# A convolution and MLP kernel whose opening is put in another order, with three accumulating transfers per tile in place of four

## The reference

```python
w = weight_gen - np.max(weight_gen, axis=-1, keepdims=True)
w = np.exp(w)
w = w / (np.sum(w, axis=-1, keepdims=True) + 1e-09)
x_pad = np.concatenate([np.zeros((B, pad, D), dtype=np.float32), x], axis=1)   # pad = 6
idx = np.arange(S)[:, None] + np.arange(K)[None, :]                            # K = 7
x_unf = x_pad[:, idx, :].reshape(B, S, K, H, group)                            # group = 24
out = np.einsum('bshk,bskhg->bshg', w, x_unf)                                  # 16384 x 192
h = out @ w_in                                                                 # 192 x 2048
g = np.maximum(0.01 * h, h)
return (g @ w_out).astype(np.float32)                                          # 2048 x 192
```

## Time and profile before

| | |
|---|---|
| median of 3 runs | 1037.89 us (1037.78 to 1038.11) |
| the profiled execution, its own time | 1039.72 us |
| its span, first to last instruction | 1037.9 us |
| PE busy with matmuls | 1026.1 us, 99% |
| DVE busy | 933.7 us, 90% |
| ACT busy | 634.8 us, 61% |
| POOL busy | 554.7 us, 53% |
| TensorE's granted clock, mean over the span | 0.997 |

### The profile page before, as it was taken

How to read it: one execution, slowest core, us unless ns; L and a number is a source line. 1 busy time by engine, 2 the same in 40 slices (tenths; PEclk the granted TensorE clock), 3 DMA queues, 4 the chain that set the end, 5 groups by cost and what they waited for, 6 DMA issues and landing times.

```text
span 1037.9 us, 28985 instructions
## 1 busy us (share of the span) xinstructions
PE 1026.1 (99%) x12761; PEld 673.6 (65%) x12761; DVE 933.7 (90%) x1196; ACT 634.8 (61%) x1352; POOL 554.7 (53%) x377
## 2 busy tenths in 40 slices
PE   9899999899999999999999999999999999999998
PEld 4566556466666666666666666666666666666667
DVE  7979999969999999999999999999999999998611
ACT  7866566465565665566565566565566565566554
POOL 0114556456566566556556556556556556556543
PEclk9999999999999999999999999999999999999999
DMA  9441212111131210312102121110312102111100
GB/s 265 102 99 32 81 35 97 34 32 66 35 96 35 59 66 8 97 35 97 34 17 81 35 97 34 50 66 17 97 34 97 34 18 81 34 35 35 34 17 17
DMA packets 68597, 60.62 MB, mean 58 GB/s; under 512 B 56380, under 2 KB 60732, under 8 KB 66488
## 3 DMA queue, kind: packets, MB, share of 16 engines
q1 hardware_dynamic: 67196, 55.35, 18.2%
q0 software_dynamic: 1152, 3.15, 1.7%
q10 hardware_dynamic: 124, 0.29, 0.1%
HBM read 29.34 MB, written 12.58 MB: 40 GB/s over the span
## 4 chain that ended last, share of the span: by engine, by line
PE 94%; DMA 2%; DVE 2%; SPq 1%; issue 0%; ACT 0%; POOL 0%; DVEq 0%; POOLq 0%
PE h_ps L1061 45%; PE t_ps L1171 23%; PE out_ps L1171 23%; PE out_ps L1125 1%; PE h_ps L1043 1%; PE out_ps L1135 1%; DMA rawD<-in_moe_w_in_dram 1%; SPq L383 1%; DMA conv<-prod 0%; DVE gl L883 0%; DMA prod<-prod 0%; SPq L386 0%; DVE prod L683 0%; PE h_ps L1099 0%; ACT gh L483 0%
## 5 line engine op out<-in xcount | busy, mean ns | idle before, releaser
L352 POOL TENSOR_TENSOR gl<-g,gh 128x512 f16<-128x512 f32 x360 | 545.6, 1542 | 413.3 <-ACT g L485 413.3
L483 ACT ACTIVATE gh<-h_ps 128x512 f16<-128x512 f32 x512 | 317.6, 620 | 373.8 <-PE h_ps L1061 362.3
L1171 PE MATMUL t_ps<-wo,gh 64*128 64x384 f16 (+1 forms) x1984 | 387.8, 318 | 4.3 <-issue 4.3
L1171 PE MATMUL out_ps<-wo,gh 64*128 64x384 f16 (+1 forms) x1984 | 387.8, 318 | 0.0
L1061 PE MATMUL h_ps<-xT,whA 64*128 64x512 f16 x1920 | 377.6, 376 | 0.0
L485 ACT ACTIVATE g<-h_ps 128x512 f32<-128x512 f32 x512 | 321.9, 629 | 0.0
L683 DVE TENSOR_TENSOR prod<-xbuf,taps 128x768 f32<-128x768 f32 x186 | 273.3, 1485 | 0.0
L697 DVE TENSOR_TENSOR conv<-conv,prod 128x768 f32<-128x768 f32 x174 | 264.5, 1520 | 1.0
L1171 PE MATMUL out_ps<-wo,gl 64*128 64x192 f16 x1920 | 233.4, 243 | 0.0
L1171 PE MATMUL t_ps<-wo,gl 64*128 64x192 f16 x1920 | 233.4, 243 | 0.0
L1171 PEld LDWEIGHTS t_ps<-wo,gh 64*128 64x128 f16 x1984 | 181.8, 94 | 51.6 <-issue 5.0
(11 more groups left out here) (111 smaller groups left out, 717.5 us busy)
## 6 DMA issues: line engine op xcount, KB each, us to landing
xbuf<-in_x_dram SPq DMA_DIRECT2D x15, 1344.0 KB, 6.0
out_dram<-stage SPq DMA_DIRECT2D x31, 384.0 KB, 2.3
taps<-in_weight_gen_dram SPq DMA_DIRECT2D x16, 224.0 KB, 5.9
xT_again<-xT SPq DMA_DIRECT2D x29, 64.0 KB, 2.1
rawO<-in_moe_w_out_dram SPq DMA_DIRECT2D x4, 384.0 KB, 9.9
conv<-prod POOLq DMA_DIRECT2D x4, 384.0 KB, 4.6
prod<-prod POOLq DMA_DIRECT2D x4, 384.0 KB, 4.4
rawA<-in_moe_w_in_dram SPq DMA_DIRECT2D x2, 512.0 KB, 8.2
```

The source lines that it names most:

```text
L352: nc.gpsimd.tensor_tensor(gl[:, q % RING, :], g[:, q % RING, :], gh[:, q % RING, :], ALU.subtract).then_inc(s_gl_p, 1)
L483: nc.scalar.activation(gh[:, q % RING, :], h_ps[q % GROUP][:], ACT.Prelu, alpha=SLOPE, scale=SHRINK0 if n < 2 * NG else SHRINK).then_inc(s ...
L1171: ins = nc.tensor.matmul(dst, a[rows, (m * NF + f) % RING, j * P:(j + 1) * P], moved, start=i == 0 and k < 2 and a is gh and f == 0 and pa ...
```

## The change

It consists of five edits.

1. **PE's opening.** `sum0` now collects in `out_ps` and `t2_ps` and the warm-up matmuls write an h bank. There are 15 + 4 of them in place of 16 + 5 + 4 + 4. The transposes of tile 0's hi follow directly on `spread_top(0)`; those of its lo stand inside `hidden_by_pe(0)`, behind the first four real matmuls.
2. **DVE's and ACT's opening.** The scale of w_in and `split_hi(("A", 0))` stand behind the lo of the first of tile 0's four rows, the other three rows' lo behind them. ACT's sums of w_out are dealt differently around its two copies out of `t_ps`. The lo of piece ("A", 1) stands ahead of the hi of ("D", 1).
3. **The load of the leftover rows** stands behind w_out's second piece.
4. **Three accumulating transfers.** The fourth (prod 1 onto conv) is gone; DVE adds prod 1 itself ("sum" 1, which waits for the first two transfers), and only "sum" 3 waits for the third.
5. **The steps of tile 1.** On DVE the sums and the scale of tile 1 stand right behind group 1; the first two softmax steps of chunk 1 stand behind `take_transposed(1)`, where they stood ahead of the sums; group 2 is two instructions; the lo of piece ("O", 3) stands ahead of `lo_of_x(1)`. On PE `project_hi(3)` stands ahead of `hidden_by_pe(1)`.

```diff
-WARM_UP = (16, 5, 4, 4)
+WARM_UP = (15, 4)
-QUEUED = [("mul", k) for k in range(7)] + [("sum", 3), ("sum", 5)] + LAST
-BOUNDED = QUEUED[:9] + [("bound", 0)] + LAST[1:]
+QUEUED = [("mul", k) for k in range(7)] + [("sum", 1), ("sum", 3), ("sum", 5)] + LAST
+BOUNDED = QUEUED[:10] + [("bound", 0)] + LAST[1:]
-        sums0 = h_ps[2:4]
+        sums0 = (out_ps[:, 0, :], t2_32_ps[:])
...
                 nc.gpsimd.dma_start(prod[:, 3, :], prod[:, 4, :], accum_op=ALU.add).then_inc(s_add_last, DMA)
-                pool.wait_ge(s_add_first, DMA * (2 * i + 1))
-                pool.wait_ge(s_add_next, DMA * (i + 1))
-                nc.gpsimd.dma_start(acc, prod[:, 1, :], accum_op=ALU.add).then_inc(s_add_first, DMA)
...
+                if n == 1:
+                    load_last_rows(sp, 1, PIECE, FF, 2)
             sp.dma_start(xbuf[:, 0, (HALO + SUB) * D:], x_rows[:, SUB * D:CHUNK * D]).then_inc(s_chunk[0], DMA)
-            load_last_rows(sp, 1, PIECE, FF, 2)
...
             hi_of_x(0)
+            abs_wo(0)
             take_transposed(0, 0)
-            abs_wo(0)
+            split_hi(("D", 0))
+            abs_wo(1)
             take_transposed(0, 1)
-            split_hi(("D", 0))
-            for n in range(1, 3):
-                abs_wo(n)
+            abs_wo(2)
...
+                    if k == 1:
+                        dve.wait_ge(s_add_first, DMA * (i + 1))
+                        dve.wait_ge(s_add_next, DMA * (i + 1))
                     if k == 3:
-                        dve.wait_ge(s_add_first, DMA * 2 * (i + 1))
                         dve.wait_ge(s_add_last, DMA * (i + 1))
...
-            def group(n):
-                dve.wait_ge(s_g, (n + 1) * GROUP)
-                at = slice(n * GROUP % RING, n * GROUP % RING + GROUP)
+            def group(n, first=0, last=GROUP):
+                dve.wait_ge(s_g, n * GROUP + last)
+                at = slice(n * GROUP % RING + first, n * GROUP % RING + last)
...
                 split_hi(("A", 1))
+                lo_pieces(2, 3)
                 split_hi(("D", 1))
-                lo_pieces(2, 4)
+                lo_pieces(3, 4)
...
                 group(1)
+                early_conv(1, ("sum", 1))
                 lo_pieces(10, 11)
+                early_conv(1, ("sum", 3), ("out_scale", 0))
+                group(2, 0, 2)
+                group(2, 2, GROUP)
+                lo_pieces(11, 12)
+                lo_of_x(1)
+                take_transposed(1)
                 dve.wait_ge(s_chunk[1], DMA * 2)
                 for n in range(2):
                     softmax(1, n)
-                early_conv(1, ("sum", 3), ("out_scale", 0))
-                group(2)
-                lo_of_x(1)
-                take_transposed(1)
-                lo_pieces(11, 12)
                 group(3)
...
-            lo_of_x(0)
+            lo_of_x(0, 0, 1)
             w_scales(0)
             split_hi(("A", 0))
+            lo_of_x(0, 1, SUB)
...
                 if m == 0:
+                    transpose_rest(0)
                     wait_piece(("A", 0))
...
                 project_lo(2)
+                wait_piece(("O", 3))
+                project_hi(3)
                 hidden_by_pe(1)
-                wait_piece(("O", 3))
-                for n in range(NG - 1, 2 * NG - 1):
+                project_lo(3)
+                hidden_early(NG + 1)
+                for n in range(NG, 2 * NG - 1):
...
-            warm_up(WARM_UP[1])
             transpose_hi(0)
-            warm_up(WARM_UP[2])
-            pe.wait_ge(s_xT_a, 1)
-            transpose_rest(0)
-            warm_up(WARM_UP[3])
+            warm_up(WARM_UP[1])
             hidden_by_pe(0)
```

More of the change, by code:

```diff
@@ L934, in second_tile @@
                 group(NG + 1)
-                early_conv(2, ("sum", 3), ("out_scale", 0))
+                early_conv(2, ("sum", 1), ("out_scale", 0))
                 group(NG + 2)
```

13 lines of the change are left out of this document (7 added, 6 removed).

## The result

The changed kernel took 1032.31 us (median of 5 runs, 1031.82 to 1036.06), the kernel before 1038.11 us beside it (1037.78 to 1039.43). The ratio is 0.9957, with a 95% interval of 0.9942 to 0.9973. Three of the five runs took 1031.82 to 1032.31 us, the other two 1035.80 and 1036.06. The profiled execution took 1031.82 us, its span 1030.0.

A forecast was written before the change was run, and what follows sets the result against it. DVE's full chain from 76 to 197 us was taken to bound the span; its gain of 5.0 gave 1039.72 − 5.0 = 1034.7 us profiled, 1037.89 − 5.0 = 1032.9 us median. Own range 1032.0 to 1033.8, wider range 1031.0 to 1035.5.

The forecast's parts named there:

- Opening: Start of the kernel: `whA` 1.35 us earlier, the second scale and DVE's group 1 1.24 us earlier.
- Tile 1, PE: PE in tile 1: waits of 1.6 and 0.5 us go, no fallen clock, group 5 starts 4.5 us earlier.
- the last sum: Closing calculation for tile 5's wait, with PE 4.6 and DVE 5.0 us earlier: 4.28 + 4.6 − 5.0 = 3.9 us.
- Tile 2, DVE: DVE's sums in tile 2: third transfer takes 4.0 us, `x_top` at 73.07 instead of 78.05, a gain of 5.0 us.
- To the end: From tile 2 to the end: DVE's 5.0 us comes through; PE's wait in tile 5 is 3.9 us, its low clock stays.
- the distance between the profile and the median: Whole kernel: the median time was taken to stand 1.8 us below the profiled execution.
- Rival C: Tile 5: wait shrinks to 3 us or less and the low clock goes; another 1.7 us gained, 1031.2 us; chance 0.08.
- the sign: Expected profile in tile 5: if DVE is early and PE's wait short, the rest of the gain came from POOL's pattern.
- Rival D: DVE's chain from 98 to 197 us lengthens as POOL slows 5 to 8 products, about 1036.7 us; chance 0.13.
- Rival A: A late link before tile 2's `x_top`, by transfer or DVE step; costs 1.1 to 1.5 us, 1034.2 us; chance 0.11.
- rival B: Opening: the clock falls with ten warm-up matmuls fewer and new waits; costs about 1.7 us, 1034.6 us; chance 0.08.

The follow-up runs named there:

- e4: The kernel before with only the new opening of PE, DVE and ACT and the moved load of the leftover rows; median 1034.80 us, ratio 0.9968.
- e2: The kernel before with twelve matmuls of zeros (2.6 us of PE) added ahead of group 8; median 1037.42 us, ratio 0.9996.
- e9: The changed kernel without the rearranged steps of tile 1, the other four edits kept; median 1034.27 us, ratio 0.9967.
- e3: The kernel before with only the three accumulating transfers and a third sum on DVE; median 1034.39 us, ratio 0.9967.
- e10: The changed kernel without the last four warm-up matmuls of the opening (15 + 0); median 1032.01 us, ratio 0.9940.
- e12: The kernel of e5 with two more matmuls of zeros on PE, which ran at 115.3 us; median 1033.73 us, ratio 0.9949.
- e1: The changed kernel run once more, unchanged, 11 runs; median 1031.91 us, ratio 0.9953 to the kernel before.
- e5: The changed kernel with two extra memsets (0.95 us) on DVE in tile 2, behind group 6; median 1036.33 us, ratio 0.9989.
- e11: The changed kernel with all `gl` of tiles 3 and 4 on POOL and block 7's `gl` ahead of the convolution in tiles 5 and 6; median 1036.82 us.
- e6: The changed kernel with POOL's `gl` over only 64 of 512 columns in tiles 2 to 5; median 1030.55 us, ratio 0.9929.

## Why the prediction was right, and where it was not

- **Opening (gain of 1.24 at group 1): right, against the profile that I read.** `whA` at 17.38 for 17.15, the second scale at 24.35 for 24.2, group 1 at 39.31 for 39.17. e4 shows this part alone. In e2's execution, the same program up to there, group 1 stands at 39.97 for 40.41, so about 0.4 of the gain is the execution.
- **Tile 1, PE (gain of 4.5; the last sum writes 4.6): right, against that profile.** Group 5 at 58.57 for 58.55 forecast. The waits of 1.6 and 0.5 us are gone and the low clock is too. But the clock does not fall in every execution that has such waits: e9 (1.26 and 0.54 us) and e2 (1.16 and 0.54) have them with a whole clock, and their group 5 starts at 60.65 and 60.67. Against those PE gains 2.1 us, and that is edit 5.
- **Tile 2, DVE (gain of 5.0): right, against that profile.** Sum 3 at 71.16, `x_top` at 73.14, 4.91 earlier. I took 4.0 us for the transfer; it took 4.1. e3 and e4 show about 2.2 and 1.8 for edit 4 and the opening; 0.85 is edit 5's, by e9. Against e2's 75.50, the kernel before without the fall, the whole gain is 2.4.
- **To the end: this step failed.** I wrote "the span ends with DVE's chain of 76 to 197", gave this chain a fixed length, and so got a wait of 4.28 + 4.6 − 5.0 = 3.9 us with its low clock. The runs show a wait of 0.9 or of 4.3 us and nothing between, in the eleven profiles that keep L777's place in DVE's row and POOL's full work, however much DVE or PE was shifted: 0.9 in the changed kernel, e2, e3, e4, e9, e10 and e12, 4.3 in the kernel before, e1, e5 and e11. DVE's lateness is a lag behind PE that POOL's batches set, not a sum of its own work. The span therefore follows PE: its gain of 4.5 comes through in either pattern, and the pattern adds or takes 3 to 4.
- **Why the number came out all the same: by luck, as far as the last step goes.** For the profiled execution I had 1034.7 us, and it took 1031.82, 2.9 less. An execution of the changed kernel in the long pattern took 1034.99 (e1), so the sum was about right for that pattern, and the 0.3 are what DVE fell short (L777 4.74 earlier than before, not 5.0). I then took off 1.8 for the distance between the profile and the median. In truth the median run of the changed kernel isn't in the pattern of the profile that I read at all: eight of e1's eleven are in the short one, 3 us below. The 1.8 happened to stand in for that, and so the forecast of 1032.9 is only 0.6 off. The runs of the kernel before reach from 1034.2 to 1043.0 us in all; 1.8 was no constant.
- **Rival C (the clock in tile 5, 0.08)** is what the changed kernel's profile shows, and for the reason named there, that DVE meets POOL less often. Its price was too small, since I counted 1.7 for the clock but not the 3.0 by which the wait is shorter than 3.9, nor the new wait of 1.35. The last section of the prediction had named the sign (a short wait, and the rest from POOL's pattern). **Rival D (0.13)** had the right mechanism too, slowed DVE work by who meets whom. I priced it as 5 to 8 slowed products with nothing that pulls DVE back. e5 shows such a meeting: 1036.33, near my 1036.7, though by one change of pattern and not by 5 to 8 products. I held a shift of 0.4 us between DVE and PE to be small. At the meeting near 111 us the two patterns lie 0.1 to 0.35 us apart.
- **Rival A (a late link)** did not occur; **rival B (the clock in the opening)** neither, and e10 shows that even the last four warm-up matmuls bought nothing. The Trainium skill's rule in "TensorE: Matmul & The Clock Gate", Part 1, "What's actually happening", that activity is what lifts the clock, is not contradicted by that, since PE had worked up to this wait of 1.06 us and went on behind it.

What stays open: why the kernel before spreads over nearly 9 us from run to run, and the changed kernel over 4. Two patterns explain 3 to 4 of it, and the fall of the clock in tile 1, which comes in some executions of the same program and not in others, some 2 more. What decides that fall, and what the runs above 1040 us met, no profile shows. No version that does all the work was clearly faster than the changed kernel; e6, which is, leaves work out.

## What to carry to other kernels

When an engine on the critical path shares a lock with one that keeps step with another engine, don't carry its lateness forward as a sum: here it settled at one of two lags, and a shift of a few tenths of a us chose which. So look at where the two start within a few tenths of a us of each other before adding up a gain, run the kernel more than ten times, and set each run's clock beside its time, before trusting a profile's wait, and count a gain of the engine that sets the step (here PE) as the safe part. Edits tried one by one don't add up where each can win the same step.
